# Moving one load, one normalisation and the masks in the attention stage of a fused attention and experts kernel

## The reference

```python
# attention: 2 batches, 8 heads, 576 positions, head size 64
scores = where(mask[head], (q @ k.T) / 8, -1e9)     # a band of 32, or every 4th of 128
attn = exp(scores - max); attn /= attn.sum(-1) + 1e-9
x = (attn @ v) as [1152 tokens, 512]
# four experts, 512 -> 1024 -> 512, weighted by the token's shares
p = probs / (probs.sum(-1) + 1e-9)
x = sum over e of p[:, e] * (relu(x @ w1[e]) @ w2[e])
# rational layer, 512 -> 2048 -> 512
h = x @ w_in
out = ((a0 + a1 h + a2 h^2 + a3 h^3) / (1 + |b0||h| + |b1| h^2 + 1e-6)) @ w_out
```

## Time and profile before

| | |
|---|---|
| runs | 673.2, 673.71, 675.17 us; median 673.71 |
| profiled execution | 675.78 us, span from first to last instruction 674.0 us |
| mean granted clock of TensorE | 0.985 |
| busy: TensorE (PE) | 654.2 us, 97% of the span |
| busy: weight loads (PEld) | 587.2 us, 87% |
| busy: VectorE (DVE), ScalarE (ACT), GpSimd (POOL) | 312.1, 303.9, 216.4 us |

### The profile page before, as it was taken

One profiled execution on the slowest core, in us unless ns is written; L12 is line 12 of the kernel. 1 busy time (PEld: TensorE's weight loads), 2 busy tenths in 40 slices (PEclk: granted clock), 3 DMA queues, 4 the chain that ended last, 5 costly groups with the idle time before them and its releaser, 6 DMA issues.

```text
span 674.0 us, 9784 instructions
## 1 busy us (share of the span) xinstructions
PE 654.2 (97%) x3716; PEld 587.2 (87%) x3716; DVE 312.1 (46%) x600; ACT 303.9 (45%) x756; POOL 216.4 (32%) x217
## 2 busy tenths in 40 slices
PE   5798999999999999999999999999999999999997
PEld 4686888899999999999999999999999999999996
DVE  7456545121212121212121212125988888889896
ACT  6785455222221122211122211225778787877773
POOL 5584122133320033320033310034642466642221
PEclk9598999999999999999999999999999999999999
DMA  8637210000330000330001420002220000001011
GB/s 321 210 129 251 66 43 1 1 1 9 133 108 0 1 1 25 131 96 1 0 1 31 126 94 1 0 1 63 94 95 1 0 2 1 0 1 48 0 48 48
DMA packets 13079, 36.83 MB, mean 55 GB/s; under 512 B 1832, under 2 KB 2856, under 8 KB 13032
## 3 DMA queue, kind: packets, MB, share of 16 engines
q1 hardware_dynamic: 13032, 36.20, 16.3%
HBM read 33.84 MB, written 2.36 MB: 54 GB/s over the span
## 4 chain that ended last, share of the span: by engine, by line
PE 91%; ACT 3%; DMA 2%; DVE 2%; issue 1%; POOLq 0%; POOL 0%; SPq 0%; DVEq 0%; ACTq 0%
PE ps_h L380 44%; PE ps_o L397 43%; DMA scratch<-in_qk_dil 2%; ACT scratch L476 2%; PE ps_a L330 1%; DVE prob_sum L690 1%; PE ps_b L357 1%; PE ps_a L342 1%; PE ps_o L357 0%; PE ps_q L342 0%; PE ps_a L418 0%; DVE scratch L654 0%; DVE acc L717 0%; ACT scratch L486 0%; PE ps_b L418 0%
## 5 line engine op out<-in xcount | busy, mean ns | idle before, releaser
L380 PE MATMUL ps_h<-x_hi,w_hi 128*128 128x384 f32 (+1 forms) x608 | 202.5, 333 | 2.6 <-DVE x_lo L682 2.6
L380 PE MATMUL ps_h<-x_hi,w_lo 128*128 128x384 f32 (+1 forms) x608 | 200.4, 330 | 0.0
L380 PE MATMUL ps_h<-x_lo,w_hi 128*128 128x384 f32 (+1 forms) x608 | 199.7, 328 | 0.0
L499 ACT ACTIVATE h_hi<-ps_h 128x384 fp32r<-128x384 f32 (+1 forms) x104 | 48.5, 467 | 292.8 <-PE ps_h L380 292.8
L702 DVE SCALAR_TENSOR_TENSOR h_lo<-ps_h,h_hi 128x384 fp32r<-128x384 f32 (+1 forms) x104 | 54.7, 526 | 271.1 <-ACT h_hi L499 271.1
L397 PE MATMUL ps_o<-w_hi,h_lo 128*128 128x512 f32 x432 | 171.3, 396 | 0.0
L397 PE MATMUL ps_o<-w_lo,h_hi 128*128 128x512 f32 x432 | 171.0, 396 | 0.0
L397 PE MATMUL ps_o<-w_hi,h_hi 128*128 128x512 f32 x432 | 169.8, 393 | 0.3 <-POOL h_lo L885 0.3
L874 POOL TENSOR_TENSOR w_lo<-raw,w_hi 128x512 fp32r<-128x512 f32 x48 | 61.8, 1288 | 214.2 <-ACT w_hi L505 213.5
L380 PEld LDWEIGHTS ps_h<-x_hi,w_hi 128*128 128x128 f32 x608 | 115.2, 189 | 10.3 <-DVE x_lo L682 2.8
L380 PEld LDWEIGHTS ps_h<-x_lo,w_hi 128*128 128x128 f32 x608 | 115.1, 189 | 5.6
(11 more groups left out here) (80 smaller groups left out, 580.6 us busy)
## 6 DMA issues: line engine op xcount, KB each, us to landing
raw<-in_weights SPq DMA_DIRECT2D x48, 512.0 KB, 3.5
scratch<-in_qk_dil SPq DMA_DIRECT2D x8, 352.0 KB, 5.3
scratch<-in_qk_plain SPq DMA_DIRECT2D x8, 304.0 KB, 5.3
out_t<-acc SPq DMA_DIRECT2D x9, 256.0 KB, 2.1
scratch<-in_v_dil SPq DMA_DIRECT2D x8, 208.0 KB
scratch<-in_v_plain SPq DMA_DIRECT2D x8, 192.0 KB, 5.1
prob<-in_probs SPq DMA_DIRECT2D x1, 18.0 KB, 14.0
a_sb<-in_a SPq DMA_DIRECT2D x1, 2.0 KB, 10.8
```

The source lines that it names most:

```text
L380: last = nc.tensor.matmul(h_of(k, f), w[:, f, dc, :], x, start=dc == 0 and i == 0, stop=dc == DC - 1 and i == 2)
L499: nc.scalar.activation(h_hi[:, s % RING, 0:ITER[k][2]], h_of(k, f), ACT.Relu).then_inc(hi_moe, 1)
```

## The change

Five edits are made.

1. `load_qk(1, 1)`, the q and k of pair 5, the sixth, is issued behind the third of the first eight weight chunks. Before, it stood behind all eight, the shares, a, b, and v of pair 4.
2. The tile of shares has a fifth column that holds 1e-9, set by VectorE at the start. The sum over five columns has the constant in it, and the separate addition goes. The load writes four of the five columns.
3. `normalise_probs` moves from block 0's last iteration to block 1's iteration with steps 2 and 3, just ahead of `take_sums` of block 0.
4. The low part of x of pair w - 1 moves behind the masks of the next iteration; before, it stood ahead of `low` of step f + 1 in its own. The last pair of each group keeps its place.
5. `normalise_probs` waits for the memset as well.

```diff
-        prob = sb("prob", [P, NT, MOE])
+        prob = sb("prob", [P, NT, MOE + 1])
...
             for c in range(FC):
                 load_raw(0, c)
-            sp.dma_start(prob[:, :, :], probs).then_inc(prob_in, 16)
+                if c == 2:
+                    load_qk(1, 1)
+            sp.dma_start(prob[:, :, 0:MOE], probs).then_inc(prob_in, 16)
...
             for pair in range(PAIRS):
-                if pair:
+                if pair > 1:
                     load_qk(1, pair)
                 load_v(1, pair)
...
             def normalise_probs():
                 dve.wait_ge(prob_in, 16)
+                dve.wait_ge(small_set, 2)
                 nc.vector.tensor_reduce(prob_sum[:, :], prob[:, :, :], axis=AX.X, op=ALU.add).then_inc(prob_step, 1)
                 dve.wait_ge(prob_step, 1)
-                nc.vector.tensor_scalar_add(prob_sum[:, :], prob_sum[:, :], 1e-9).then_inc(prob_step, 1)
+                nc.vector.reciprocal(prob_sum[:, :], prob_sum[:, :]).then_inc(prob_step, 1)
                 dve.wait_ge(prob_step, 2)
-                nc.vector.reciprocal(prob_sum[:, :], prob_sum[:, :]).then_inc(prob_step, 1)
-                dve.wait_ge(prob_step, 3)
-                nc.vector.tensor_tensor(prob[:, :, :], prob[:, :, :],
+                nc.vector.tensor_tensor(prob[:, :, 0:MOE], prob[:, :, 0:MOE],
                                         prob_sum[:, :].unsqueeze(2).to_broadcast([P, NT, MOE]), ALU.mult)\
                     .then_inc(prob_step, 1)
-                dve.wait_ge(prob_step, 4)
+                dve.wait_ge(prob_step, 3)
...
             nc.vector.memset(row_sum[:, :, :, 1], 1e-9).then_inc(small_set, 1)
+            nc.vector.memset(prob[:, :, MOE], 1e-9).then_inc(small_set, 1)
...
                     if more:
                         mask(2 * w + 2)
                         mask(2 * w + 3)
+                    if f:
+                        attention_lo(w - 1)
...
                     if more:
                         invert(2 * w + 3)
+                    if k == 1 and f == LAG - 1:
+                        normalise_probs()
                     if k and f == LAG - 1:
                         take_sums(k - 1)
-                    if k == 0 and f == FC - 2:
-                        normalise_probs()
-                    attention_lo(w)
+                    if f == FC - 2:
+                        attention_lo(w)
                     if k or f >= LAG:
                         low(k, f + 1)
```

## The result

| | before | after |
|---|---|---|
| median of 5 runs | 673.83 us (673.2 to 675.17) | 666.51 us (665.84 to 666.75) |
| profiled execution, span | 675.78, 674.0 us | 666.47, 664.7 us |
| mean granted clock | 0.985 | 0.991 |

The ratio of after to before, taken from the means of the runs, is 0.9887, with a 95% interval of 0.9873 to 0.9902: faster by 7.6 us, 6.6 to 8.6. The two medians lie 7.3 us apart. The forecast was 664.8 us in a range of 662.9 to 667.4. The time lies in the range, 1.7 us above the forecast.

What follows compares the result with a forecast made beforehand. TensorE bounds the kernel: nothing behind about 73 us can be shortened by reordering, so its earlier waits count. 1.94 + 0.2 + 0.9 + 6.6 − 0.74 = 8.9 us off the 673.71 median gives 664.8 us, range 662.9 to 667.4.

Steps and rivals of the forecast that it cites:

- The load: Before `scores(5)`: q/k of the sixth pair issued earlier, landing before 20, ends TensorE's wait; gain 1.94 us, clock 0.2.
- The masks: Before `turn(5)`: masks 12 and 13 ahead of low parts of x cut TensorE's 1.06 us wait; gain 0.9 us.
- the 3.04 of the sum: Gains up to the transposes of pair 5: 1.94 and 0.2 from the early load, 0.9 from the masks.
- the 0.15 of the text: Wait of TensorE for masks expected to be left before `turn(5)`, down from 1.06 us.
- The 0.2 us for the clock: Opening stage at clock 0.50: one TensorE pause fewer before full clock returns; 0 to at most 1.05, taken as 0.2.
- The shares: Pair 8's step without L688 to L694: 14.46 becomes 7.86 us, gain 6.6, less 0.74 stall at the new place.
- the two values for the product: Stall before the first `take_sums`: 0.74 us if product L694 is held by GpSimd's L858, 0.2 if not; 0.74 taken.
- The rule on two SBUF inputs: VectorE instruction with two SBUF inputs contends with a GpSimd one reading SBUF; by it the sum has 0.74, otherwise 0.2.
- Rival 2: L690's 4.66 us is the first TENSOR_SCALAR's price and passes to L712; gain 1.7, time 672.0; chance 0.04, with similar ones.
- Rival 1: Early load's gain is eaten by ScalarE's queue order, 30 to 37 us; 666.9 us; chance 0.18, including other partial losses.
- Rival 3: Shares' 16-byte pieces delay the seventh pair's load; at 240 ns each 675.8 us; chance 0.03, including an unseen stall.

Runs made afterwards that it cites:

- the quieter base: The kernel after, run again unedited beside the last variants on one chip: 666.57 us; without the masks' edit it took 667.48 us there.

## Why the prediction was right

**The load** was sized at 1.94 + 0.2 us and measured 2.1 alone. It was issued at 7.36 (forecast 7.6), landed 8.9 us later at most, by 16.3 (forecast before 20), and the wait went.

**The masks** were sized at 0.9 and measured 0.9, on the quieter base. Up to the transposes of pair 5 the sum held in total: 37.63 − 34.13 is 3.50, less 0.28 by which this execution's first load came sooner, 3.2 against the 3.04 of the sum. The wait left over is 0.5, not the 0.15 of the text. By the same reckoning VectorE's masks started 3.2 us sooner (forecast 3.04), but TensorE was ready for the transposes 2.7 us sooner (forecast 2.14); its clock had come back in the 29th microsecond, not the 33rd. The 0.2 us for the clock can't be told apart from the rest. It was a choice between 0 and 1.05. Two traces of the kernel after, with clocks of 0.72 and 1.00 over 14 to 32 us, start the transposes 30.58 and 30.02 us after their first matmul, which points to some 0.6 us for the clock in this kernel, an estimate from two executions.

**The shares** were sized at 6.6 − 0.74 = 5.9 and measured 4.85 alone, inside an interval of 3.6 to 6.1. The mechanism was as forecast: the step of pair 8 became 7.84 us. Of the two values for the product the held one came true (0.57 us in the trace; the step of pair 9 is 0.79 us longer, where the stall was put at 0.74), and so the choice made from rows was right. The rule on two SBUF inputs of the Trainium skill, page "SBUF — State Buffer", section "Who interferes with whom", which the prediction cited, agrees with the trace of after (0.57 us).

**The 1.7 us by which the forecast is low.** Between the two profiled executions the sum came true nearly term by term: 3.48 us ahead of pair 8's step, 6.62 in it, −0.79 in the next, together 9.3 for a forecast of 8.9 (675.78 to 666.47; the prediction had 666.9 by this count). Between the medians only 7.3 us were gained. So the slip is one that the text named and then made: before's profiled execution was 2.1 us above the median, and its gain was carried into the median unchanged. Which term is smaller in a usual execution is not settled. TensorE's stops for the addition are alike in all four traces that have it in its old place (2.5 to 2.6 and 0.5 to 0.7 us), but the time at the low clock level behind them was 6.8 us in three and 3.4 in one, and the step took 14.46, 14.27, 14.38 and 13.10 us. The wait for the sixth pair's load was 1.94 us in the trace that the sum is made from, and 1.78 and 1.24 in two others. What a low execution of before (671.5 us) looks like was not seen.

**Rival 2** (the first TENSOR_SCALAR) is refuted by the addition at 0.82 us. **Rival 1** is refuted by the load alone. **Rival 3** (the 16-byte pieces) looked for the price in the wrong place: it shows at SP's issue, where the next load stood 7.1 and 8.8 us. It was covered all the same: the seventh pair's load was issued at 21.20 and landed 5.9 us later, at 27.1, where before it landed at 27.6.

**What the text didn't see.** It read the 6.6 us rightly as what the step saves once L688 to L694 are gone from it, all four of them, and charged 0.74 for the new place. What it didn't see is how the two edits share this. The move alone earns it: with the addition kept the time is the same (666.40). Removing the addition without the move loses 3.5 of the 7.6 us, since the product, the next instruction that needs GpSimd out of the way, stalls in its place (670.04). Edit 2, the fifth column, was not needed.

## What to carry to other kernels

When a small instruction of VectorE takes microseconds, look at what GpSimd does until the moment it ends. Taking that instruction away can pass its stall on to the next one of its group. Move the whole group to a place where GpSimd is idle or has one short instruction, best where VectorE waits anyway; here the gap ahead of `low` was 0.7 to 1.2 us better than just ahead of the first `take_sums`. A stall that drops TensorE's clock costs a different amount in each execution, so a gain read from one execution should be subtracted from that execution, or be compared with the spread of the runs first, and a small edit should be measured on the kernel whose runs spread least.

## What the runs showed of the hardware

A VectorE product with two SBUF inputs (128x36) took 0.20 us with GpSimd idle, 0.57 and 0.62 against one GpSimd instruction, and 4.34 against four in a row. An addition with one SBUF input (128x9) took 0.82 and 0.87 us against one GpSimd instruction, and 4.66 against four in a row. A reciprocal of the same 128x9 that came 0.06 us after the start of GpSimd's L864 took 0.21 and was not held. Whether the product could get in between two of them, had there been a gap, was not tried. The Trainium skill, page "SBUF — State Buffer", section "Who interferes with whom", has the loser wait for the whole instruction of the one that came first; the 4.34 us are more than that, a whole row of instructions. So are the addition's 4.66 us in the kernel before, which the prediction took as plain agreement: L858, the one that had come first, ended 0.85 us after the addition came.

A load of 18 KB in rows of 16 bytes was itself issued in 0.65 us (0.45 in rows of 144 bytes), but the next load on the same queue then stood 8.8 us in SP, and 7.1 to 9.4 in five other traces. In the two kernels that have the early load and four columns it stood 0.43 us. With the 16-byte rows issued late, at 24.58 us, the load behind them took 1.02 us.
